# Attention with two fused layers on one NeuronCore: the second layer step of a slot ahead of its first transposes, with edits to staging, layer product and tail scores

## The reference

```python
def _attn_ref(q, k, v):                       # (4, 8, 576, 64) each
    scores = 1/sqrt(64) * np.matmul(q, k.transpose(0, 1, 3, 2))
    kth = np.partition(scores, -32, axis=-1)[..., -32:-31]
    scores = np.where(scores >= kth, scores, -1e9)
    attn = np.exp(scores - np.max(scores, axis=-1, keepdims=True))
    attn = attn / (np.sum(attn, axis=-1, keepdims=True) + 1e-09)
    return np.matmul(attn, v)

def _moe_ref(x, w_in, w_out):                 # first layer
    h = x @ w_in
    g = np.where(h >= 1, h, np.where(h <= -1, 0.0, (h + 1) ** 2 / 4))
    return g @ w_out

def _moe2_ref(x, w_in, w_out):                # second layer
    h = np.maximum(x @ w_in, 0.0)
    return h * h @ w_out
```

## Time and profile before

| | |
|---|---|
| time, median of 3 runs | 1233.21 us (1232.77 to 1233.88) |
| the profiled execution: its own time | 1234.77 us |
| the profiled execution: span of its instructions | 1233.0 us |
| mean granted TensorE clock | 0.977 of full speed |
| busy: TensorE, VectorE, ScalarE, GpSimd | 1181.6, 836.8, 778.2, 740.8 us |

### The profile page before, as it was taken

The page is one execution under the profiler, slowest core; times in us unless marked ns, Lnnn a source line. Parts: engine busy times, 40 slices in busy tenths (PEclk is TensorE's granted clock), DMA queues, the critical chain, the costliest instruction groups (busy, mean ns, idle before and its releaser), DMA issues.

```text
span 1233.0 us, 23032 instructions
## 1 busy us (share of the span) xinstructions
PE 1181.6 (96%) x8184; PEld 1096.6 (89%) x8184; DVE 836.8 (68%) x1863; ACT 778.2 (63%) x1672; POOL 740.8 (60%) x589
## 2 busy tenths in 40 slices
PE   5878899999999999999999999999999999999998
PEld 3767888999889999999999999999999888998887
DVE  7999999999987799899999987878740111110000
ACT  6896666787765767767776665666654544653343
POOL 5786876888977767777676766665652222222222
PEclk9867999999999999999999999999999999999999
DMA  7776796778869932433458831466439500780000
GB/s 254 284 273 229 276 348 231 267 248 308 327 225 396 390 106 99 141 109 135 138 191 302 292 118 39 141 188 191 125 132 373 188 1 1 314 335 1 1 35 18
DMA packets 94914, 239.45 MB, mean 194 GB/s; under 512 B 7760, under 2 KB 46672, under 8 KB 82512
## 3 DMA queue, kind: packets, MB, share of 16 engines
q1 hardware_dynamic: 94640, 237.71, 54.0%
q10 hardware_dynamic: 160, 0.26, 0.1%
HBM read 166.12 MB, written 71.83 MB: 193 GB/s over the span
## 4 chain that ended last, share of the span: by engine, by line
PE 73%; DVE 8%; POOL 8%; ACT 5%; issue 3%; DMA 2%; SPq 0%; ACTq 0%; POOLq 0%
PE h_ps L694 22%; PE y_ps L728 10%; PE y_ps L722 10%; PE pv_ps L653 6%; PE score_ps L694 6%; DVE top L1060 4%; DVE rest L1062 3%; PE tr_ps L626 3%; PE score_ps L591 3%; POOL s_sb L1239 3%; POOL prob L1244 2%; PE y_ps L714 2%; PE y_ps L717 2%; PE tr_ps L714 2%; PE tr_ps L717 2%
## 5 line engine op out<-in xcount | busy, mean ns | idle before, releaser
L694 PE MATMUL h_ps<-xt_ks,w_in 128*128 128x256 f32 (+1 forms) x2628 | 386.2, 297 | 1.7 <-ACT rg L934 1.0
L694 PEld LDWEIGHTS h_ps<-xt_ks,w_in 128*128 128x128 f32 x2628 | 343.2, 191 | 11.9 <-ACT rg L934 1.4
L1257 POOL TENSOR_TENSOR g_lo<-rg,g_hi 128x256 fp32r<-128x256 f32 x224 | 169.4, 756 | 284.2 <-ACT g_hi L952 165.5
L1060 DVE MAX8 top<-rest 128x8 f32<-128x576 f32 x432 | 304.3, 745 | 0.4
L1239 POOL TENSOR_SCALAR s_sb<-s_sb,top 128x576 f32<-128x576 f32 x126 | 221.8, 1760 | 33.3 <-DVE top L1060 33.3
L1062 DVE MATCH_REPLACE8 rest<-top,rest 128x576 f32<-128x576 f32 x288 | 211.3, 740 | 0.0
L1244 POOL TENSOR_TENSOR prob<-s_sb,prob 128x576 f32<-128x576 f32 x128 | 183.0, 1432 | 16.8 <-DVE top L1060 3.8
L722 PE MATMUL y_ps<-g_hi,w_out 128*128 128x256 f32 x896 | 180.8, 285 | 1.2 <-POOL g_lo L1257 0.8
L728 PE MATMUL y_ps<-w_out,g_hi 128*128 128x512 f32 x448 | 158.6, 395 | 0.8 <-ACT moves L913 0.7
L722 PEld LDWEIGHTS y_ps<-g_hi,w_out 128*128 128x128 f32 x896 | 147.5, 192 | 3.2 <-POOL g_lo L1257 1.8
L653 PE MATMUL pv_ps<-v_sb,pt 128*128 128x65 f32 x1024 | 132.4, 287 | 0.0
(11 more groups left out here) (122 smaller groups left out, 1871.2 us busy)
## 6 DMA issues: line engine op xcount, KB each, us to landing
w_in<-w_scratch SPq DMA_DIRECT2D x32, 1024.0 KB, 6.7
w_out<-w_scratch SPq DMA_DIRECT2D x32, 1024.0 KB, 8.0
xt_ks<-kq_scratch SPq DMA_DIRECT2D x46, 576.0 KB, 6.1
qs_g<-kq_scratch SPq DMA_DIRECT2D x152, 128.0 KB, 4.1
w_scratch<-w_in SPq DMA_DIRECT2D x16, 1024.0 KB, 7.2
w_scratch<-w_out SPq DMA_DIRECT2D x16, 1024.0 KB, 6.8
v_sb<-in_vv_dram SPq DMA_DIRECT2D x48, 325.0 KB, 5.8
moves<-in_w_dram SPq DMA_DIRECT2D x27, 512.0 KB, 6.8
```

Source lines behind the costliest of these rows:

```text
L694: last = pe.matmul(h_bank(k), wi[:, f // 2, w, m, cols], x_part(k, x, m), start=(m == 0 and n == 0), stop=(m == KT - 1 and n == 2))
L1060: dve.max(best, src[:, :]).then_inc(rank_step, 1)
L1257: pool.tensor_tensor(lo_of(k), u_of(k), hi_of(k).bitcast(F32), ALU.subtract).then_inc(g_lo_done, 1)
```

## The change

It has four parts.

- **Staging.** Weight blocks 4 to 10 are staged at the end of slots 0, 0, 0, 1, 2, 2 and 3, after the next `load_kq`, where they stood in slots 0, 1, 1, 2, 3, 3 and 4 ahead of it.
- **Layer product.** In slots 10 to 17 `up` of position 3n + 3 is issued in slot n already, ahead of `times_v`.
- **Tail scores.** The packed units take three products of parts instead of four. The two heads lie stacked in the 128 rows, so a unit has 6 matmuls of 288 columns where it had 10 matmuls with 2304 columns in all, and five smaller DMAs load it where three did.
- **The second step.** From slot 18 on `at(3n + 1)` stands ahead of `turn_main(n - 1, 0)`. ScalarE's `copy_at(q)` moves ahead of `copy_main(n - 1, 0)`, which shows in slots 24, 40 and 62.

```diff
-STAGE_SLOT = [-1, -1, -1, -1] + [s + 1 for s in W_SLOT[0:12]] + [16, 16, 18] + [s - 1 for s in W_SLOT[19:]]
+STAGE_SLOT = [-1, -1, -1, -1] + [max(s, 0) for s in W_SLOT[0:7]] + [s + 1 for s in W_SLOT[7:12]] + [16, 16, 18] + [s - 1 for s in W_SLOT[19:]]
+AHEAD = 11
...
+            def load_tail(g, i):
+                sp.wait_ge(restacked, 16 * 3 * (PREP_ORDER.index(g) + 1))
+                heads = kq_dram[g][0:2, :, :].rearrange("x (d h) c -> h d x c", h=2)
+                for h, to, cols in ((0, slice(0, SEQ), slice(0, SEQ)),
+                                    (1, slice(0, MAIN), slice(TAIL, SEQ)),
+                                    (1, slice(MAIN, SEQ), slice(0, TAIL))):
+                    sp.dma_start(ks[i][DIM * h:DIM * (h + 1), :, to].bitcast(F32), heads[h, :, :, cols]
+                                 ).then_inc(ks_loaded[i], 16)
+                for h in range(2):
+                    sp.dma_start(qs[i][DIM * h:DIM * (h + 1), 0, :, :].bitcast(F32),
+                                 heads[h, :, :, SEQ + P * (QT - 1):KQ]).then_inc(qs_loaded[i], 16)
...
-                load_ks(e, e % 2)
-                load_qs(e, QT - 1, e % 2)
+                load_tail(e, e % 2)
...
-                for i in range(4, WBLOCKS):
+                for i in range(AHEAD, WBLOCKS):
                     if STAGE_SLOT[i] == n:
                         stage_block(i)
...
                 at(3 * n + 2)
-                for i in range(WBLOCKS, 2 * WBLOCKS):
+                for i in (*range(4, AHEAD), *range(WBLOCKS, 2 * WBLOCKS)):
                     if STAGE_SLOT[i] == n:
                         stage_block(i)
...
-                    for var in range(2):
+                    for i, (x, y) in enumerate(((0, 0), (0, 1), (1, 0))):
                         for half in range(2):
-                            pe.matmul(score_ps[:, 512 * half:512 * half + HALF], qq[:, 0, var, :],
-                                      kk[:, 0, HALF * half:HALF * (half + 1)],
-                                      start=(var == 0), stop=False, skip_group_check=True)
...
+                            last = pe.matmul(score_ps[:, 512 * half:512 * half + HALF], qq[:, 0, x, :],
+                                             kk[:, y, HALF * half:HALF * (half + 1)],
+                                             start=(i == 0), stop=(i == 2))
...
+            def up_ahead(q):
+                if q in UP_AT and q // 3 - 1 in SINGLE:
+                    up(UP_AT[q])
...
-                if k is not None:
+                if k is not None and not (q % 3 == 0 and q // 3 - 1 in SINGLE):
                     up(k)
...
                 if n + 1 < SLOTS:
                     score(n + 1, 0)
+                if n >= DEFERRED[0]:
+                    at(3 * n + 1)
                 if 0 <= n - 1 < SLOTS:
                     turn_main(n - 1, 0)
-                at(3 * n + 1)
+                if n < DEFERRED[0]:
+                    at(3 * n + 1)
...
                 at(3 * n + 2)
+                up_ahead(3 * n + 3)
...
                     copy_scores(n + 1, 0)
+                copy_at(q)
                 if before:
                     copy_main(n - 1, 0)
-                copy_at(q)
```

More of the change, by code:

```diff
@@ L595, in score @@
                     e = 2 * (n - NORMAL) + t
-                    pe.wait_ge(ks_loaded[t], 16 * (NORMAL // 4 + e // 2))
+                    pe.wait_ge(ks_loaded[t], 16 * (NORMAL // 4 - 1 + 3 * (e // 2 + 1)))
                     pe.wait_ge(qs_loaded[t], 16 * 2 * (NORMAL // 2 + e // 2 - 1))
                     kk, qq = ks[t], qs[t]
-                    for var in range(2):
+                    for i, (x, y) in enumerate(((0, 0), (0, 1), (1, 0))):
                         for half in range(2):
-                            pe.matmul(score_ps[:, 512 * half:512 * half + HALF], qq[:, 0, var, :],
-                                      kk[:, 0, HALF * half:HALF * (half + 1)],
-                                      start=(var == 0), stop=False, skip_group_check=True)
[L604 to L611, removed]
+                            last = pe.matmul(score_ps[:, 512 * half:512 * half + HALF], qq[:, 0, x, :],
+                                             kk[:, y, HALF * half:HALF * (half + 1)],
+                                             start=(i == 0), stop=(i == 2))
                 last.then_inc(scored, 1)
```

## The result

The changed kernel takes **1289.76 us** (median of 4 runs, 1289.14 to 1290.37); the kernel before, beside it on the same chip, 1233.55 (1232.77 to 1234.78). The ratio is 1.0455, with a 95% interval of 1.0437 to 1.0473: 56 us slower. The profiled execution has a span of 1287.4 us at a mean granted clock of 0.984.

What follows compares the result with a forecast made beforehand. TensorE, busy 1181.6 of 1233.0 us, was taken as the bound. 48.4 + 15.2 - 5 + 5 - 5.8 - 3 = +54.8 on 1234.8 gave 1289.6, less 1.6 for the median: 1288 us, range 1260 to 1306.

Steps and rivals of the forecast that it cites:

- The step ahead of the transposes: Slots 18 to 49 and 51 to 62: up waits 1.1 us a slot for ScalarE's relu, 44 slots, +48.4 us.
- P: The first start of unit 0's transposes on TensorE in a slot; up of step 3n+2 forecast at P + 2.52 us.
- The tail: Slots 63 to 72: the same wait, 1.6 us in slots 64 to 70, together +15.2 us.
- What it gives back: TensorE's 4.1 us of waits for GpSimd's masked probabilities go, and about 1 us of others: -5 us.
- Job starts: Token splits and output copies in slots 23, 39, 61, 29, 45, 67 and 44 add +5 us, between 0 and 9.
- Tail scores: Packed tail score units take 0.80 us instead of 1.16, 16 x 0.36 = -5.8 us.
- Layer product: Slots 10 to 17: earlier up cuts VectorE's idle times, -3 us, bounds 0 and -3.8.
- Staging: Slots 0 to 4: weight blocks loaded up to a slot earlier, 0 us, between -1 and +2.
- The sum: All terms together: +54.8 us on the profiled execution's 1234.8, so 1289.6, and 1288 us for the median.
- B: Rival: VectorE paces the slots with weight splits, 18 to 34; 18.7 us less, 1269 us; chance 0.12.
- C: Rival: TensorE doesn't wait, the copy chain being shorter than what it issues; only gains left, 1219 us; chance 0.07.
- D: Rival: TensorE's added idle time brings back stretches at half clock; +25 us, 1313 us; chance 0.08.

Runs made afterwards that it cites:

- copy_behind_exp: Changed kernel with, from slot 18 on, ScalarE's copy of unit 0's transposes moved behind exp of unit 1; 1252.87 us.
- copy_behind_ghi: Changed kernel with, from slot 18 on, ScalarE's copy of unit 0's transposes behind exp and g_hi, right ahead of step 3n+1; 1240.42 us.
- step_undone: Changed kernel with the second step and ScalarE's output copy put back where they were, the other three parts kept; 1224.03 us, in a second series 1223.22.
- quiet_only: relu_first, but slots 18, 22, 23, 34, 39, 50, 51, 56, 61 and those from 71 on keep the old orders; 1225.74 us.
- tail_alone: Kernel before with only the tail scores of three products; 1229.82 us, ratio 0.9958.
- staging_alone: Kernel before with only the earlier staging of weight blocks 4 to 10; 1233.42 us, ratio 0.9992.
- step_alone: Kernel before with only the second step moved ahead of the transposes, and ScalarE's output copy with it; 1297.02 us, ratio 1.0526.
- relu_first: Changed kernel with, from slot 18 on, ScalarE's copy of unit 0's transposes behind the relu and squares of step 3n+1; 1231.35 us.
- third_up_ahead: step_undone with up of step 3n+2 ahead of unit 1's transposes from slot 19 on, not at a job's first step; 1244.90 us.

## Why the prediction was right, point by point

**The step ahead of the transposes (forecast +48.4).** Right in mechanism and size. The chain from the transposes to `up` was forecast at P + 2.52 and measured at P + 2.52; the slot at 13.78. Slots with three steps and nothing else grew by 1.11. Slot 51, one of the 44, did not grow at all, and slot 50, which has one step and was not counted, grew by 1.3; the two cancel. The piece of the estimate that mattered was taken from the one place of the trace before where the same chain already decided, slot 51. copy_behind_exp and copy_behind_ghi show that it is this chain, by taking its links out.

**The tail (+15.2).** Against step_undone slots 63 to 72 grew by 14.7 us: 1.6 to 1.7 in slots 64 to 70 but for 67, which had a wait to share and grew by 1.1; 0.9, 2.3 and 0.8 in slots 63, 71 and 72 for a forecast 0.8, 2.4 and 0.9.

**What it gives back (-5).** The sum was nearly right, its reason was not. "The 4.1 us of waits for GpSimd go": by the idle times on TensorE's timeline from slot 19 on, unit 0's waits went (5 times, 3.2 us in before), but unit 1's grew from 2 times and 0.9 us to 16 times and 10.0, because the second transposes are reached with the mask of unit 1 not done. In a steady slot that cost nothing on top: in slots 20 and 21 TensorE idles 0.44 us ahead of the second transposes and only 0.22 ahead of `up`, and the slot is still 13.78. What did come off is that the new wait swallowed old ones: slots 25, 27, 28, 30, 32 and 51 grew by only 0 to 0.8 us against step_undone, together 4.1 us less than 1.1 each. And in quiet_only, without the queue fault, the earlier step gives back nothing that shows.

**Job starts (+5, between 0 and 9).** Against step_undone slots 23, 24, 29, 34, 39, 40, 44, 45, 48, 56 and 61 grew by 1.1 and another 5.7 us in all. That this is near 5 is in part luck: the six of them that the forecast named (23, 29, 39, 44, 45, 61) give 3.1 us, 67 gives nothing, and 2.7 come from five that it didn't name. The mechanism was half of it. TensorE does wait for the output copy, 0.6 us of idle time in 24 and 29 and 1.0 in 45. But in slots 23, 34, 39, 45, 48, 50, 56 and 61 a `down` also waits for GpSimd's low part, 0.4 to 1.4 us (the longest in 61), where step_undone has that in 39 alone, 0.3 us. This is the second wait that the prediction checked in slot 36 with "It holds": it holds in steady slots, and not in loaded ones. The 50.2 us of slots 19 to 62 are 43 x 1.1 + 5.7 + 1.3 - 4.1, to the rounding.

**Tail scores (-5.8).** Measured 5.8 us over slots 63 to 72, and 5.2 by the times of tail_alone. That this is the forecast to the decimal is luck. Steady tail slots give 0.85 us for two units, 0.43 each for the 0.36 of the rows, but slot 67 gives nothing and slot 68 only 0.6. The score units did shrink as forecast, from 1.16 to 0.79 and 0.80 us; the 0.06 beyond that lie behind them, where the transposes take 0.36 and 0.46 us to the next `up` in slot 64 of tail_alone for 0.41 and 0.52 in before. An estimate by the columns alone, as the Trainium skill's "TensorE: Matmul & The Clock Gate", section "Wait — 56ns, not 53.3ns?", counts them, was 0.25 us a unit and 4.0 in all; the measured 0.43 and 5.8 lie above it, and the trace decides.

**Layer product (-3, bound -3.8).** The sign and the stretch were right, the bound was wrong: 4.4 us at slot 19. The step of the argument that failed is the ceiling. It counted VectorE's two largest idle times; the small ones, 0.9 us in 45, went as well. Nor was the largest, 2.18 us, simply a late `up`. It stands behind the stretch at half the clock; TensorE and ScalarE of before there:
```profile
164.08 0.46 PE L648 MATMUL pv_ps<-v_sb,pt 128*128 128x130 f32 x2 [1.46 <-ACT pt L857]
166.65 2.67 PE L694 MATMUL h_ps<-xt_ks,w_in 128*128 128x256 f32 x12
169.35 0.39 ACT L939 ACTIVATE rg<-h_ps 128x256 f32<-128x256 f32 x1 [4.46 <-PE h_ps L694]
```
All four kernels profiled without the early `up` (before, tail_alone, staging_alone, step_alone) have one such fall between 142 and 167 us, 1.3 to 1.7 us behind a wait of the product with v for pt of 1.4 to 1.6 us, and VectorE's long wait follows it: 2.18, 2.17, 2.35 and 2.25 us. Where the clock fell at 142 or 143, VectorE has no such wait at 170. None of the nine profiled executions with the early `up` has such a wait for pt or a fall between 126 us and slot 19. So some 2 of the 4.4 us came with the clock, which the forecast didn't put into this term. No run changed the clock alone, so this rests on the order of events in thirteen profiled executions.

**Staging (0).** Right by the time. In the one profiled execution it is a sum of two effects that were not in the forecast: what it gains until slot 19 is spent again by slot 24.

**The sum.** The profiled executions differ by 54.4 us for a forecast 54.8, and that is closer than the parts. Up to slot 19 the forecast had -1.9 (layer product and slot 18's wait) and -4.4 was measured; for slots 19 to 62 it had +47.3 and +49.8 was measured; for slots 63 to 72 +9.4 and +9.0. Two misses of 2.5 us cancel.

**The rivals.** B, VectorE paces slots 18 to 34, is refuted: those slots grew by 1.1 like the others where they had no wait of their own. C is refuted by the waits for the relu in 50 slots. D is refuted for this kernel; from slot 18 on the granted clock stays at full:
```profile
214.00:500.00 286.00, 266.87 (x1995) 248.79 (x1994) 230.52 (x510) 182.67 (x408) 210.92 (x156) 1.00 0.68 250
500.00:740.00 240.00, 222.89 (x1814) 214.84 (x1813) 203.04 (x456) 154.09 (x362) 154.30 (x122) 1.00 0.48 166
740.00:960.00 220.00, 201.30 (x1413) 184.51 (x1413) 163.60 (x382) 125.08 (x301) 133.64 (x122) 1.00 0.42 112
```
TensorE idles 7 to 9% of these stretches in after, the waits for the relu in pieces of 0.2 to 0.9 us and, in the tail, of 1.3 to 1.6.

## What to carry to other kernels

When one engine's in-order queue is reordered, look at the other engines' queues for an instruction that waits for the moved work and stands ahead of something that is ready: what stands between the two in that queue sets the new wait. Cost the chain from a place where the trace shows the same chain already deciding, and shorten it link by link to prove it. A step whose latency was already hidden gained nothing here by moving earlier, while the masks and copies that it was moved ahead of came around later, and the slots with extra work paid for that first.

## What was not expected of the hardware

The granted clock fell to 0.50 for some 3.3 us behind single waits of 1.8 and 2.6 us of TensorE in two experiments, while the waits for the relu in the changed kernel, idle times of up to 0.9 us and in the tail of 1.3 to 1.6, left it at 1.00. The length of a wait doesn't tell alone: in relu_first one of 1.71 us at 270.6 us left the clock at 1.00 where one of 1.78 didn't, and in before one of 1.46 us was followed by a fall and one of 1.6 ahead of it wasn't. Ahead of the first, TensorE was busy 5.77 of 8 us; ahead of the second 7.42 of 8 between 262 and 270 us (third_up_ahead):
```profile
262.00:270.00 8.00, 7.42 (x62) 7.21 (x62) 8.00 (x19) 6.73 (x14) 7.92 (x5) 1.00 0.68 232
```
So one long wait cost more than its length (2.91 us for 1.67 us of matmuls), and many short ones did not. What decides between them these runs don't show. And GpSimd's first masking instruction took 2.95 to 3.15 us for 1.72 in slots 22 and 23 of several kernels, without a cause that these runs name.
